# Four up-weight sums per group moved from GpSimd to VectorE, in two halves, in a fused attention and two-MLP kernel

## The reference

```python
kv  = einsum('bhsd,bhse->bhde', k, v)            # attention without softmax, 8 heads of 64
out = einsum('bhsd,bhde->bhse', q, kv)
x   = out / sqrt(mean(out*out, -1) + 1e-6) * g_norm
u   = x + (x^T @ U @ V)^T                        # rank 32 over the tokens
x2  = u + relu(u @ w_ch1) @ w_ch2                # 512 -> 2048 -> 512
h   = gelu(x2 @ w_in)                            # 512 -> 1024, halves u, v
out = x2 + (u * (w_sg @ layernorm(v) + b_sg)) @ w_out
```

## Time and profile before

| what | us |
|---|---|
| three runs | 1255.78, 1254.95, 1254.92 |
| median | 1254.95 |
| the profiled execution, its own time | 1254.6 |
| its span, first to last instruction | 1253.0 |
| PE busy | 1234.6 (99%) |
| DVE busy | 926.4 (74%) |
| ACT busy | 575.4 (46%) |
| POOL busy | 109.4 (9%) |
| granted PE clock, mean | 0.999 |

### The profile page before, as it was taken

One profiled execution on the slowest core, in us unless ns is written; L12 is line 12 of the kernel. 1 busy time (PEld: TensorE's weight loads), 2 busy tenths in 40 slices (PEclk: granted clock), 3 DMA queues, 4 the chain that ended last, 5 costly groups with the idle time before them and its releaser, 6 DMA issues.

```text
span 1253.0 us, 21860 instructions
## 1 busy us (share of the span) xinstructions
PE 1234.6 (99%) x8129; PEld 1194.3 (95%) x8129; DVE 926.4 (74%) x1380; ACT 575.4 (46%) x942; POOL 109.4 (9%) x123
## 2 busy tenths in 40 slices
PE   7999999999999999999999999999999999999998
PEld 6899999999999999999999999999898998998987
DVE  5987677676757678988888989987865656558564
ACT  4674555554545546554544545544333333343330
POOL 5430000000000000000000000001120211221100
PEclk9999999999999999999999999999999999999999
DMA  9788878878787677473553637362242251350421
GB/s 213 186 215 209 207 198 221 217 206 204 200 218 213 177 246 280 146 259 119 184 173 129 208 126 259 109 181 81 58 91 78 53 117 50 71 122 28 97 59 42
DMA packets 364840, 195.87 MB, mean 156 GB/s; under 512 B 259776, under 2 KB 334800, under 8 KB 364768
## 3 DMA queue, kind: packets, MB, share of 16 engines
q1 hardware_dynamic: 360480, 189.77, 54.4%
q0 software_dynamic: 1728, 4.57, 1.5%
q10 hardware_dynamic: 2560, 0.59, 0.2%
HBM read 118.19 MB, written 74.58 MB: 154 GB/s over the span
## 4 chain that ended last, share of the span: by engine, by line
PE 93%; DVE 4%; DMA 1%; issue 1%; ACT 0%; SPq 0%; POOL 0%; DVEq 0%; POOLq 0%; ACTq 0%
PE ps L1772 28%; PE ps L1774 28%; PE ps L1773 28%; PE ps L1793 3%; PE ps L1804 2%; PE ps L1812 1%; PE ps L2089 1%; PE ps L2092 1%; DVE w L1286 1%; PE ps L1830 1%; PE ps L1777 1%; DMA q_raw<-in_q 1%; PE ps L1806 0%; DMA v_raw<-in_v 0%; DVE y L1242 0%
## 5 line engine op out<-in xcount | busy, mean ns | idle before, releaser
L1772 PE MATMUL ps<-x_hi,w 128*128 128x288 f32 x896 | 267.8, 299 | 2.1 <-DVE x_lo L1315 0.9
L1773 PE MATMUL ps<-x_lo,w 128*128 128x288 f32 x896 | 264.2, 295 | 0.0
L1774 PE MATMUL ps<-x_hi,w 128*128 128x288 f32 x896 | 263.9, 295 | 0.0
L1772 PE MATMUL ps<-r_hi,w_hi 128*128 128x384 f32 x672 | 224.6, 334 | 0.4 <-DVE r_lo L1497 0.4
L1774 PE MATMUL ps<-r_hi,w_lo 128*128 128x384 f32 x672 | 224.5, 334 | 0.0
L1773 PE MATMUL ps<-r_lo,w_hi 128*128 128x384 f32 x672 | 224.5, 334 | 0.0
L1091 ACT ACTIVATE r_hi<-hb 128x768 fp32r<-128x768 f32 x168 | 142.3, 848 | 166.4 <-PE ps L1774 161.1
L1772 PEld LDWEIGHTS ps<-x_hi,w 128*128 128x128 f32 x896 | 168.1, 188 | 4.3 <-DVE h_st L1326 1.4
L1774 PEld LDWEIGHTS ps<-x_hi,w 128*128 128x128 f32 x896 | 168.6, 188 | 0.0
L1773 PEld LDWEIGHTS ps<-x_lo,w 128*128 128x128 f32 x896 | 168.4, 188 | 0.0
L1499 DVE TENSOR_TENSOR r_lo<-hb,r_hi 128x768 fp32r<-128x768 f32 x120 | 114.6, 957 | 30.7 <-ACT r_hi L1091 30.7
(11 more groups left out here) (196 smaller groups left out, 2539.4 us busy)
## 6 DMA issues: line engine op xcount, KB each, us to landing
hT_scratch<-h_st SPq DMA_DIRECT2D x64, 576.0 KB, 4.2
hb<-hT_scratch SPq DMA_DIRECT2D x24, 1536.0 KB, 7.2
uT_scratch<-x_raw SPq DMA_DIRECT2D x32, 288.0 KB, 4.6
x_st<-uT_scratch SPq DMA_DIRECT2D x24, 384.0 KB, 3.6
x2T_scratch<-x_st SPq DMA_DIRECT2D x24, 384.0 KB, 5.6
x_raw<-x2T_scratch SPq DMA_DIRECT2D x16, 576.0 KB, 4.1
xt_in<-x2T_scratch SPq DMA_DIRECT2D x144, 64.0 KB, 2.6
y_scratch<-y SPq DMA_DIRECT2D x26, 320.0 KB, 3.2
```

Of the source, the lines that this page charges most:

```text
L1772: mm(dst, ws[0], xs[0], start=first, stop=False, skip_group_check=chained)
L1773: mm(dst, ws[0], xs[1], start=False, stop=False, skip_group_check=chained)
L1774: return mm(dst, ws[1], xs[0], start=False, stop=last, skip_group_check=chained)
```

## The change

The sums of groups 2 and 3 are taken from POOL and given to DVE. `w1_sums` gets a parameter `part`: 0 issues the first two instructions, 1 the last two. In group g (1 and 2) of tile 0, DVE does part 0 of group g + 1 at `at_` 8, directly behind the split of a, and part 1 at `at_` 9, behind the `added` of that step. ACT's high halves move from `at_` 7 and 9 to 10 and 11, so behind the low-rank evacuation; DVE's low halves from 10 and 12 to 12 and 13. POOL's DMAs of group 3 now wait for DVE's sums of group 2. POOL gets one wait more, late in the program, for its own early memsets.

```diff
-        def w1_sums(eng, ops, g):
+        def w1_sums(dve, g, part=None):
             raw = w1_raw[min(g, 1)][:, max(0, 2 * g - 2):max(2, 2 * g), 1]
-            eng.wait_ge(s_w1[g], 16 * 8)
-            ops.tensor_tensor(raw[:, :, 1], raw[:, :, 4], raw[:, :, 6], ALU.add).then_inc(s_wsum[g], 1)
-            ops.tensor_tensor(raw[:, :, 4], raw[:, :, 0], raw[:, :, 4], ALU.subtract).then_inc(s_wsum[g], 1)
-            eng.wait_ge(s_wsum[g], 1)
-            ops.tensor_tensor(raw[:, :, 2], raw[:, :, 1], raw[:, :, 0], ALU.subtract).then_inc(s_wsum[g], 1)
-            eng.wait_ge(s_wsum[g], 3)
-            ops.tensor_tensor(raw[:, :, 5], raw[:, :, 3], raw[:, :, 2], ALU.subtract).then_inc(s_wsum[g], 1)
+            if part != 1:
+                dve.wait_ge(s_w1[g], 16 * 8)
+                nc.vector.tensor_tensor(raw[:, :, 1], raw[:, :, 4], raw[:, :, 6], ALU.add).then_inc(s_wsum[g], 1)
+                nc.vector.tensor_tensor(raw[:, :, 4], raw[:, :, 0], raw[:, :, 4], ALU.subtract).then_inc(s_wsum[g], 1)
+            if part != 0:
+                dve.wait_ge(s_wsum[g], 1)
+                nc.vector.tensor_tensor(raw[:, :, 2], raw[:, :, 1], raw[:, :, 0], ALU.subtract).then_inc(s_wsum[g], 1)
+                dve.wait_ge(s_wsum[g], 3)
+                nc.vector.tensor_tensor(raw[:, :, 5], raw[:, :, 3], raw[:, :, 2], ALU.subtract).then_inc(s_wsum[g], 1)
...
             load_w1(2, slice(4, 6))
-            pool.wait_ge(s_wsum[1], 4)
-            for g in range(2, NG):
-                pool.wait_ge(s_p, 2 * NI * (g - 2) + 4)
-                w1_sums(pool, nc.gpsimd, g)
-                if g == 2:
-                    load_w1(3, slice(6, NPAIR))
+            pool.wait_ge(s_wsum[2], 4)
+            load_w1(3, slice(6, NPAIR))
...
+            pool.wait_ge(s_zero, 3 * HP + 7)
             inverse_std(0, 0)
...
-            W1_HIGH_AT = (LOW, LOW + 2)
+            W1_HIGH_AT = (LOW + 3, LOW + 4)
...
-            W1_LOW_AT = (LOW + 3, LOW + 5)
+            W1_LOW_AT = (LOW + 5, LOW + 6)
...
                     if first and k == LOW + 2:
-                        w1_sums(dve, nc.vector, 1)
+                        w1_sums(dve, 1)
+                    if first and 0 < g < NG - 1 and LOW < at_ < LOW + 3:
+                        w1_sums(dve, g + 1, at_ - LOW - 1)
```

More of the change, by code:

```diff
@@ L1370, in _ @@
                 if m == 1:
-                    w1_sums(dve, nc.vector, 0)
+                    w1_sums(dve, 0)
                 elif m > 1:
```

## The result

| | before | changed |
|---|---|---|
| median of 6 runs, us | 1254.97 | 1263.63 |
| lowest to highest | 1254.92 to 1258.49 | 1262.29 to 1264.45 |
| the profiled execution | 1254.6 | 1264.45 |
| its span | 1253.0 | 1262.8 |

The ratio is 1.0062, 95% interval 1.0049 to 1.0074: slower by 8.7 us by the medians, where the forecast was 4.5 slower (1259.4, range 1256.8 to 1261.5). The direction was right, the size missed by a factor of two, and the time lies outside the range.

A forecast was written before the change was run, and what follows sets the result against it. PE, busy for 1234.6 of 1253.0 us, was taken as the bound, so only its waits count. Terms -1.61 + 1.75 - 0.26 + 3.8 + 0.8 = +4.5 us gave a median of 1259.4, range 1256.8 to 1261.5.

The forecast's parts named there:

- step 1: Sums leaving POOL end its stretching of DVE, removing PE's waits for y's low part: -1.61 us group 1, -0.26 group 2.
- steps 2 and 3: Group 1: weight chain behind a's split readies the second low half L + 11.05 (L: low-rank products' start); PE loses +1.75 us.
- step 4: Group 2: transpose of y and completion of u precede the second low half, ready at L + 12.6; +3.8 us.
- step 5: Group 3's DMAs, ACT's later copies and squares, and POOL's new wait cost nothing; DMAs have 2.3 us of cover.
- the largest term of the forecast: Group 2: PE begins the second step of group 3 later against the low-rank products' start, +3.8 us.
- more than the sum: Rival: group 3's DMAs land over 2.3 us late, or clock stays low a second stretch; 1261.5 or more, chance 0.08.
- step 6: PE's clock falls behind group 2's waits of 1.3 and 2.7 us: between 0 and +1.5 us, taken as +0.8.
- the rival of full clock: Rival: the same PE waits for weights but no fall of the clock, +3.7 us, 1258.6; chance 0.27.
- The rival on the other side: Rival: weights always in time in both groups, only POOL's contention counts, -1.87 us, 1253.1; chance 0.05.

The follow-up runs named there:

- experiment 4: Kernel before with POOL's eight sums of groups 2 and 3 replaced by six memsets, so weights differ: 1254.95 us, ratio 0.9985.
- experiment 1: Changed kernel with tile 0's low part of the next tile's first x block moved from k = 33 to k = 44: 1261.83 us, ratio 1.0036.
- experiment 3: Changed kernel with DVE's second low half in group 2 of tile 0 ahead of the transpose of y and completion of u: 1262.11 us, ratio 1.0039.
- changed, again: The changed kernel itself, run once more on another chip: 1263.38 us, ratio 1.0059.
- experiment 2: Changed kernel with POOL issuing group 3's weight DMAs after 20 PE steps instead of behind DVE's sums of group 2: 1262.46 us, ratio 1.0040.
- experiment 5: Kernel before, sums still on POOL, with the change's new places for high halves (10, 11) and low halves (12, 13): 1261.24 us, ratio 1.0053.
- 6: Changed kernel with the moves of experiment 1, experiment 2 and experiment 3 together: 1258.79 us, ratio 1.0027.
- experiment 10: Changed kernel with only the high and low halves of groups 2 and 3 made in two pieces each: 1258.22 us, ratio 1.0016.
- experiment 7: Changed kernel with the moves of experiment 1 and experiment 2, and halves of groups 2 and 3 in two pieces each: 1256.33 us, ratio 1.0002.
- 8: As experiment 7, with the first two sums at place 5, where DVE is idle, and the last two directly behind the split: 1255.40 us, ratio 0.9994.
- 11: As 8, with group 3's sums at places 1 and 5 and `x_low` at k = 38: 1254.48 us, ratio 0.9991.

## Why the prediction was wrong

**Right, within 0.1 us:** POOL's sums gone, -1.61 in group 1 (step 1 of the forecast, and experiment 4); the chain behind the split of a, L + 11.08 for L + 11.05, and so +1.75 (steps 2 and 3); the chain of group 2 without the late transfer, 12.61 for 12.6 (step 4 and experiment 1). Of step 4 the share of the transpose and the completion of u, 1.5 to 1.6 us, measured 1.46 (experiment 3).

**Wrong, step 5: "What else moves, at nothing".** I asked of the moved weight DMAs only whether they themselves land in time, and gave them 2.3 us of cover. They do land in time: DVE never waits for them. But they moved to where another transfer begins, the store of `x_raw`, whose landing DVE awaits in program order ahead of the split of a. In the same step I let ACT's copies come later because the sum of squares behind them stands late anyway; but SP's stores wait for these copies too, and the same store is queued behind them. The store takes 2.5 us longer and comes 0.4 later, and DVE, rid of the stretching that step 1 counts as pure gain, asks for it 0.9 sooner, against 0.4 us of slack; DVE waits 3.49, and the largest term of the forecast becomes +6.52 instead of +3.8. The trace of the kernel before showed the risk: the store landed 0.4 us ahead of the moment when DVE came to `x_low`; I did not list what `x_low` waits for. Of the rivals "more than the sum" came nearest, at 0.08. Its first cause, the DMAs of group 3 landing late, is not what happened; its second, a clock that stays low for a second stretch, did happen in the profiled execution and is 2.0 of its 9.8 us.

**Wrong in size, step 6: the clock, +0.8.** That it falls behind a wait of 2.4 us was right, and the rival of full clock fell. I took 1.5 us as the upper bound from 3.0 us of a low stretch that is 3.4 long in the trace, and took it that there is one such stretch at most. The low stretch of the changed kernel lasts 6.8 us and costs 2.83. Over the executions with a profile:

| kernel | L to second step of group 3 | waits for the low halves of group 3 | clock 0.50 for | seven steps behind |
|---|---|---|---|---|
| before | 8.79 | none | none | 5.60 |
| changed | 15.31 | 1.03, 2.42 | 6.8 | 8.43 |
| changed, again | 16.03 | 0.33, 2.42 | 3.4 | 7.10 |
| 1 | 12.61 | 1.03, 2.42 | 6.8 | 8.13 |
| 2 | 13.01 | 1.02, 2.42 | 6.8 | 7.96 |
| 5 | 11.48 | none, 2.42 | 3.4 | 7.21 |
| 3 | 13.85 | 1.03, 0.87 | none | 5.70 |
| 6 | 11.08 | 1.03, 0.88 | none | 5.78 |

With the wait of 2.42 us the clock falls in five executions of five, whether or not a shorter wait stands ahead of it, and costs 1.5 to 1.6 us (3.4 us low) or 2.4 to 2.8 (6.8 low); with waits of 1.03 and 0.9 it does not, in two of two. The three that are low for 6.8 us are those with a wait of 1.0 ahead of the 2.42, too few to make a rule of it. Nor is there a border in the length of a wait: in experiment 10 the clock fell behind 1.64 and 0.60, in the changed kernel it did not behind 1.67 and 0.60. I had cited the Trainium skill ("TensorE: Matmul & The Clock Gate", section Part 1: The HAM clock gate) for a watch on activity with a clock of its own, so that where the fall lies varies. The traces agree: against the end of the 2.42 us wait, the fall lies between 1.7 us ahead (experiment 2, at 92.5) and 0.6 us behind (experiment 5, at 93.8). What I drew from it, that the kernel with such a wait should scatter more, they do not show: the changed kernel's six runs spread over 2.2 us, those of the kernel before over 3.6.

**The rival on the other side,** weights always in time, was no outcome of this change, but experiments 7, 8 and 11 made it: with the weights in pieces the waits go, and the kernel comes near to where that rival put it: +0.2 to +0.6 us in experiment 7, -0.3 to -0.8 in 8 and -1.1 to -1.3 in 11 (by ratio or by medians), against -1.9.

**What stays open:** how the store's lateness divides in executions with no profile, since it took 8.6 and 9.3 us in the two seen; what makes the low stretch 3.4 or 6.8 us long; and the 0.66 us of the start, which differs from one execution to the next in all kernels.

## What to carry to other kernels

When transfers or copies move, list for each transfer already in flight there who waits for its landing, and what stands behind that waiter in its engine's fixed order; whether the moved one itself lands in time is only half of the question. If weights are made just in time, look which part of them the first products need: two pieces took away four waits of 4.9 us that no reordering had removed. And a short wait of TensorE may be dear: one of 2.4 us cost 1.5 to 2.8 us more by the clock behind it. Last, an engine made faster asks sooner: DVE came 0.9 us earlier to a transfer for which it had 0.4 us of slack.

## What the runs showed of the hardware

- A store of 288 KB, issued by SP, took 6.1 to 6.3 us from issue to landing in five executions in which the eight weight loads of 128 KB had been issued 3.5 us earlier or more (before, experiments 2, 4, 5 and 6), and 7.8 to 9.3 in four in which the last of them was issued in the same microsecond (changed twice, experiments 1 and 3). With the weights in pieces it was 4.6 to 5.5 (experiments 7, 8 and 11) against 6.9 (experiment 10).
- The granted clock went to 0.50 behind a wait of 2.42 us in five executions of five, for 3.4 us in two and 6.8 in three, though PE worked in 6.1 of the 6.8. After waits of 1.03 and 0.9 it stayed at 1.00 in two of two. Behind 1.64 and 0.60 it fell (experiment 10), behind 1.67 and 0.60 it did not (changed).
- While POOL made sums with operands in SBUF, DVE's low half of 128x1024, a subtraction of two SBUF operands, took 2315 ns instead of 1217; beside POOL's memsets it took 1220 (experiment 4).
